# Bonus of the first two chunks through TensorE, the state update behind the values, decay copies on ScalarE

## What is computed

```python
cur = np.einsum('bhd,bhe->bhde', u[None] * kt, vt)
y[:, :, t] = np.einsum('bhd,bhde->bhe', rt, state + cur)
state = wt[:, :, :, None] * state + np.einsum('bhd,bhe->bhde', kt, vt)
```

## Time and profile before

| | |
|---|---|
| median of three runs | 666.23 us |
| the profiled execution | 666.1 us, of which 664.3 us are the traced span |
| TensorE busy | 655.3 us (99%), 4683 matmuls |
| VectorE, ScalarE, GpSimd busy | 402.5, 218.3, 243.1 us |
| chain that ended last | 90% TensorE |
| granted TensorE clock | full in every slice of the page |
| first real product of the dense layer (step 0) | 19.95 us |

### The profile page before, as it was taken

How to read it: one execution, slowest core, us unless ns; L and a number is a source line. 1 busy time by engine, 2 the same in 40 slices (tenths; PEclk the granted TensorE clock), 3 DMA queues, 4 the chain that set the end, 5 groups by cost and what they waited for, 6 DMA issues and landing times.

```text
span 664.3 us, 12577 instructions
## 1 busy us (share of the span) xinstructions
PE 655.3 (99%) x4683; PEld 600.0 (90%) x4683; DVE 402.5 (61%) x750; ACT 218.3 (33%) x447; POOL 243.1 (37%) x293
## 2 busy tenths in 40 slices
PE   9999999999999999999999999999999999999998
PEld 6888899877878888899999999999999999999997
DVE  7888888766644333656565656565656565656563
ACT  3673434434335444422222222222222222222221
POOL 4888332222014069996006940008920009000000
PEclk9999999999999999999999999999999999999999
DMA  9913322220000032300002200003200011001011
GB/s 338 405 78 126 107 104 86 84 84 1 1 1 1 4 95 92 96 1 1 1 1 95 96 1 0 0 5 104 83 1 0 0 48 49 0 1 47 0 48 48
DMA packets 12862, 38.81 MB, mean 58 GB/s; under 512 B 1552, under 2 KB 3344, under 8 KB 12816
## 3 DMA queue, kind: packets, MB, share of 16 engines
q1 hardware_dynamic: 12528, 37.77, 16.4%
q10 hardware_dynamic: 288, 0.39, 0.2%
HBM read 35.80 MB, written 2.36 MB: 57 GB/s over the span
## 4 chain that ended last, share of the span: by engine, by line
PE 90%; DVE 6%; ACT 1%; issue 1%; POOL 0%; DMA 0%; DVEq 0%; ACTq 0%; POOLq 0%
PE bank L1029 29%; PE bank L1030 28%; PE bank L1031 28%; PE bank L919 2%; DVE fr L628 1%; DVE fr L636 1%; PE bank L976 1%; PE bank L945 1%; DVE w_lo L720 1%; PE bank L931 1%; PE bank L988 1%; DVE bank L755 0%; DMA rkw<-rkw_dram 0%; DVE x_lo L712 0%; DVE g_lo L761 0%
## 5 line engine op out<-in xcount | busy, mean ns | idle before, releaser
L1029 PE MATMUL bank<-x_lo,w_hi 128*128 128x256 f32 (+2 forms) x432 | 146.9, 340 | 1.7 <-DVE x_lo L712 0.9
L1031 PE MATMUL bank<-x_hi,w_hi 128*128 128x256 f32 (+2 forms) x432 | 143.3, 332 | 0.0
L1030 PE MATMUL bank<-x_hi,w_lo 128*128 128x256 f32 (+2 forms) x432 | 143.2, 331 | 0.0
L1030 PE MATMUL bank<-w_hi,g_lo 128*128 128x384 f32 x384 | 129.6, 338 | 0.0
L1031 PE MATMUL bank<-w_hi,g_hi 128*128 128x384 f32 x384 | 129.3, 337 | 0.0
L1029 PE MATMUL bank<-w_lo,g_hi 128*128 128x384 f32 x384 | 129.0, 336 | 0.0
L581 ACT ACTIVATE g_hi<-bank 128x512 fp32r<-128x512 f32 x96 | 57.6, 600 | 144.2 <-DVE bank L850 122.2
L1029 PEld LDWEIGHTS bank<-x_lo,w_hi 128*128 128x128 f32 x432 | 81.2, 188 | 13.0 <-issue 1.8
L1031 PEld LDWEIGHTS bank<-x_hi,w_hi 128*128 128x128 f32 x432 | 81.2, 188 | 9.0
L1030 PEld LDWEIGHTS bank<-x_hi,w_lo 128*128 128x128 f32 x432 | 81.3, 188 | 8.2
L417 POOL TENSOR_TENSOR raw<-raw 128x128 f32<-128x128 f32 x16 | 7.5, 467 | 200.5 <-DMA raw<-w_dram 200.5
(11 more groups left out here) (98 smaller groups left out, 1134.4 us busy)
## 6 DMA issues: line engine op xcount, KB each, us to landing
raw<-w_dram SPq DMA_DIRECT2D x48, 384.0 KB, 3.8
rkw<-rkw_dram SPq DMA_DIRECT2D x10, 772.5 KB, 4.5
tok<-tok_dram SPq DMA_DIRECT2D x12, 576.0 KB, 4.1
out_dram<-acc SPq DMA_DIRECT2D x10, 192.0 KB, 1.9
rkw<-rkw_dram SPq DMA_DIRECT2D x2, 512.0 KB, 4.5
rkw<-rkw_dram SPq DMA_DIRECT2D x2, 260.5 KB, 3.4
out_dram<-acc ACTq DMA_DIRECT2D x2, 192.0 KB, 2.0
u_rep<-u_dram SPq DMA_DIRECT2D x1, 192.0 KB, 6.3
```

Of the source, the lines that this page charges most:

```text
L1029: pe.matmul(out, wh, ml, start=start, stop=False, skip_group_check=shared)
L1030: pe.matmul(out, wl, mh, start=False, stop=False, skip_group_check=shared)
L1031: return pe.matmul(out, wh, mh, start=False, stop=stop, skip_group_check=shared)
```

## The change

For chunks 0 and 1 the token form of r and k is not loaded. ScalarE copies the unscaled k (d by token) into the unused part of `tok` and writes r·u into `ru`, four activations of 128 columns with a column of u as scale. GpSimd (chunk 0) and VectorE (chunk 1) multiply the two, and TensorE sums over d by four matmuls of 128 columns of weights with a two-column matrix of ones. VectorE multiplies v by these sums for both chunks. `scale_k` and `scale_r` of the two chunks now wait for ScalarE's copies. The column form of u (`u_col`) is loaded by two DMAs of single floats, ahead of the second chunk's decays; u by row moves behind the first eight slices.

`update(c)` of chunks from 2 on moves to the end of step 4c+2, behind the values, with its sums in bank 7; `add_update(c)` moves into step 4c+3, ahead of `scale_r(c+1)`. The scores of a chunk now wait for the update of the chunk before. The `tail` copy goes to ScalarE. At the start `turn_bonus(0)` moves ahead of `update(0)`, and `lo_w(0, 1)` behind both `lo_x`.

```diff
+TAILS = ALPHAS | {FIRST: INVERSES[FIRST] + 1}
-        BESIDE = dict(x=bank[6:8], yt=bank[5], kt=bank[5], u=heads_in(bank[5], 0))
+        BANKS0 = dict(x=bank[6:8], ..., bonus=bank[3])
+        BESIDE = dict(x=bank[6:8], yt=bank[5], kt=bank[5], u=heads_in(bank[7], 256))
 @block.sync
             load_decays(0)
             load_rk(0)
+            sp.wait_ge(s_zero, 1)
+            for o in range(2):
+                u_heads = bass.AP(u_d.tensor, o * D, [[1, D], [PD, PAIRS]])
+                sp.dma_start(u_col[64 * o:64 * o + D, :], u_heads, ...).then_inc(s_uc, 16)
             load_decays(1)
...
-            load_tok(0)
+            load_v(0)
+            load_v(1)
+            load_slices(0, 1, 2, 3, 4, 5, 6, 7)
             sp.dma_start(u_rep[:, :], u_d).then_inc(s_u, 16)
 @block.gpsimd
             pool.wait_ge(s_f, FIRST)
+            pool.wait_ge(s_kc, 1)
+            pool.wait_ge(s_ru, PAIRS)
+            pool.tensor_tensor(ru[:, 0, :], ru[:, 0, :], kc_of(0), ALU.mult).then_inc(s_ruk[0], 1)
             pool.wait_ge(s_qp, FIRST)
-            ... (the products of r, k, u and bonus_v of the first two chunks)
 @block.scalar
+            def copy_tail(c):
+                act.wait_ge(s_f, c + 1)
+                need(act, s_al, c - 1)
+                act.copy(tail[:, c % 2, :], fr[:, 2 * SEG - 1:SCAN:2 * SEG]).then_inc(s_tail, 1)
+            def raw_rk(c):
+                act.wait_ge(s_rkw[c], 16)
+                act.copy(kc_of(c), k_of(c)).then_inc(s_kc, 1)
+                act.wait_ge(s_uc, 32)
+                for p in range(PAIRS):
+                    cols = slice(p * CH, (p + 1) * CH)
+                    act.activation(ru[:, c, cols], q_of(c)[:, cols], ACT.Copy, scale=u_col[:, p:p + 1]).then_inc(s_ru, 1)
+            copy_tail(0)
+            raw_rk(0)
+            raw_rk(1)
+            copy_tail(1)
             copy_kt(0, BANKS0)
 @block.vector
             scale_r(1)
-            dve.tensor_tensor(tok[0][:, 0:DM], tok[0][:, 0:DM], u_rep[:, :], ALU.mult).then_inc(s_ru, 1)
-            bonus(0)
+            dve.tensor_tensor(ru[:, 1, :], ru[:, 1, :], kc_of(1), ALU.mult).then_inc(s_ruk[1], 1)
+            bonus_v(0, BANKS0)
             mask_scores(1, 0, BANKS1)
             mask_scores(1, 1, BANKS1)
-            bonus(1)
-            bonus_v(1)
+            bonus_v(1, BANKS1)
             lo_w(0, 0)
-            lo_w(0, 1)
             lo_x(0, BANKS0["yt"])
             lo_x(1, BANKS1["yt"])
+            lo_w(0, 1)
...
-                for c in due(n, 4):
-                    if c < NUPDATE:
-                        add_update(c, BESIDE)
                 elu(n)
...
+                for c in due(n, 3):
+                    if c < NUPDATE:
+                        add_update(c, BESIDE)
                 for c in due(n, 0, PRODUCTS):
 @block.tensor
 scores:         pe.wait_ge(s_x, FIRST)
+                    pe.wait_ge(s_sum, 2 * min(c, NUPDATE))
 update:
-                if banks is BESIDE:
-                    pe.wait_ge(s_x, c + 1)
+            def bonus(c, banks):
+                pe.wait_ge(s_ruk[c], 1)
+                if c == 1:
+                    pe.wait_ge(s_kt, 1)
+                for p in range(PAIRS):
+                    ins = pe.matmul(banks["bonus"][:, 2 * p:2 * p + 2], ru[:, c, p * CH:(p + 1) * CH], ones[:, :],
+                                    start=True, stop=True)
             fill(3, 1)
+            bonus(0, BANKS0)
             fill(1, 2)
             values(0, BANKS0["yt"])
             fill(5, 1)
             scores(1, BANKS1)
+            bonus(1, BANKS1)
             turn_k(1, BANKS1)
+            turn_bonus(0, BANKS0["yt"], False)
             update(0, BANKS0)
             fill(1, 4)
             values(1, BANKS1["yt"])
-            turn_bonus(0, BANKS0["yt"], False)
             turn_bonus(1, BANKS1["yt"], False)
...
                     values(c, BESIDE["yt"])
-                for c in due(n, 3):
                     if c < NUPDATE:
                         update(c, BESIDE)
```

More of the change, by code:

```diff
@@ L134, in bass_linear_attention_elu_ffn_dense_experts @@
             u_rep = sb("u_rep", [P, DM], scope=scope)
+            u_col = sb("u_col", [P, PAIRS], scope=scope)
+            ones = sb("ones", [P, 2], scope=scope)
+            ru = sb("ru", [P, FIRST, NRK], scope=scope)
             bonus_sb = sb("bonus_sb", [P, 2, H], scope=scope)
@@ L164, in heads_in @@
             return b[:, first:first + PAIRS * D]
-        BANKS0 = dict(x=bank[6:8], yt=bank[2], kt=bank[5], u=heads_in(bank[6], 0))
-        BANKS1 = dict(x=bank[0:2], yt=bank[4], kt=bank[7], u=heads_in(bank[7], 0))
-        BESIDE = dict(x=bank[6:8], yt=bank[5], kt=bank[5], u=heads_in(bank[5], 0))
+        BANKS0 = dict(x=bank[6:8], yt=bank[2], kt=bank[5], u=heads_in(bank[6], 0), bonus=bank[3])
+        BANKS1 = dict(x=bank[0:2], yt=bank[4], kt=bank[7], u=heads_in(bank[7], 0), bonus=bank[5])
+        BESIDE = dict(x=bank[6:8], yt=bank[5], kt=bank[5], u=heads_in(bank[7], 256))
         s_const = sem("s_const")
@@ L186, in bass_linear_attention_elu_ffn_dense_experts @@
         s_rk = sem("s_rk")
+        s_uc = sem("s_uc")
+        s_kc = sem("s_kc")
         s_ru = sem("s_ru")
+        s_ruk = [sem(f"s_ruk{i}") for i in range(FIRST)]
+        s_pb = sem("s_pb")
         s_bon = sem("s_bon")
@@ L282, in rk_done, with kc_of @@
         def rk_done(c):
-            return 3 + 4 * (c - 1)
+            return 4 * (c - 1)
+        def kc_of(c):
+            return tok[c][:, 0:NRK]
         def column_halves(first):
@@ L338, in load_rk, with load_v @@
                 sp.dma_start(rkw[c][:, 0:2 * NRK], rkw_d[c][:, 0:2 * NRK]).then_inc(s_rkw[c], 16)
+            def load_v(c):
+                sp.dma_start(tok[c][:, 2 * DM:3 * DM], tok_d[c][:, 2 * DM:3 * DM]).then_inc(s_tok[c], 16)
             load_decays(0)
             load_rk(0)
+            sp.wait_ge(s_zero, 1)
+            for o in range(2):
+                u_heads = bass.AP(u_d.tensor, o * D, [[1, D], [PD, PAIRS]])
+                sp.dma_start(u_col[64 * o:64 * o + D, :], u_heads, allow_slow_non_contiguous=True).then_inc(s_uc, 16)
             load_decays(1)
@@ L371, in _ @@
         def _(pool):
+            pool.memset(u_col[:, :], 0.0).then_inc(s_zero, 1)
             pool.memset(st[:, :, :, :], 0.0).then_inc(s_zero, 1)
@@ L376, in _ @@
             pool.memset(v_odd[:, :, :, :], 0.0).then_inc(s_zero, 1)
+            pool.memset(ones[:, :], 0.0).then_inc(s_zero, 1)
+            for o in range(2):
+                pool.wait_ge(s_zero, 6 + o)
+                pool.memset(ones[64 * o:64 * o + D, o:o + 1], 1.0).then_inc(s_zero, 1)
+            pool.wait_ge(s_zero, 8)
             pool.memset(credit[:, 2:3], 0.0).then_inc(s_down, RING)
@@ L566, in _ @@
                     copy_odd(c)
+                for c in due(n, 1, TAILS):
+                    copy_tail(c)
                 if n % J1 == LAG - 1 and n > LAG:
@@ L641, in alphas @@
             def alphas(c):
[L643 to L649, removed]
+                first_half = fr[:, SEG - 1:SCAN:2 * SEG]
+                need(dve, s_st, c - 3)
+                dve.wait_ge(s_tail, c - 1)
+                dve.tensor_tensor(alpha[:, c % 2, :], tail[:, c % 2, :], first_half, ALU.mult).then_inc(s_al, 1)
             def scale_k(c):
@@ L654, in scale_k @@
                 landed(dve, s_rkw, c)
+                if c < FIRST:
+                    dve.wait_ge(s_kc, c + 1)
                 dve.tensor_tensor(halves(k_of(c)), halves(k_of(c)), factors(0, SCAN + SEG + 1),
@@ L693, in bonus, with bonus_v @@
             def bonus(c):
[L695 to L699, removed]
+                dve.wait_ge(s_rk, rk_done(c))
+                dve.wait_ge(s_cv, c - 1)
                 dve.tensor_reduce(bonus_sb[:, c % 2, :], tok[c % DEEP][:, 0:DM].rearrange("p (h d) -> p h d", h=H),
                                   AX.X, ALU.add).then_inc(s_bon, 1)
-            def bonus_v(c):
-                dve.wait_ge(s_bon, c + 1)
+            def bonus_v(c, banks):
+                dve.wait_ge(s_pb, c + 1)
+                landed(dve, s_tok, c)
                 dve.tensor_tensor(bonus_v_sb[:, c % 2, :].rearrange("p (h e) -> p h e", h=H),
                                   v_of(c).rearrange("p (h e) -> p h e", h=H),
-                                  bonus_sb[:, c % 2, :].unsqueeze(2).broadcast_to([P, H, D]),
+                                  banks["bonus"][:, 0:H].unsqueeze(2).broadcast_to([P, H, D]),
                                   ALU.mult).then_inc(s_cv, 1)
@@ L926, in turn_k @@
                     pe.wait_ge(s_x, c)
-                    pe.wait_ge(s_sum, 2 * c)
                 k = k_of(c)
@@ L962, in turn_bonus @@
                     pe.wait_ge(s_x, c)
-                    pe.wait_ge(s_sum, 2 * min(c, NUPDATE))
                 for k in range(KT):
@@ L1012, in _ @@
             fill(3, 1)
+            pe.wait_ge(s_zero, 8)
+            bonus(0, BANKS0)
             fill(1, 2)
```

31 lines of the change are left out of this document (11 added, 20 removed).

## The result

The changed kernel takes 667.94 us (median of 10 executions, 667.89 to 668.33), the kernel before beside it 666.17 (10 executions, 666.01 to 666.51). The ratio is 1.0027, with a 95% interval of 1.0018 to 1.0035: 1.77 us slower. The profiled execution took 667.93, with a span of 666.1 us where before it was 664.3. The forecast was 667.1.

The account below looks back on a forecast made before the run. TensorE, busy 99% of the span, was taken as the bound, with ScalarE and VectorE pacing the first steps. Start +2.3 and chunks -1.3 gave +1.0 on 666.1, so 667.1 us, range 664.0 to 669.4.

Parts of the forecast that it names:

- `u_col`, 0.2 late: Start: the single-float loads land at 5.9 us, ScalarE's activations end at 7.1, so `scale_r(0)` starts 0.2 us late.
- Rival C: Start: `u_col` lands two microseconds behind 5.9, everything behind it goes later, total 669.1 us; chance 0.14.
- The bonus, 0.9 each: Start, TensorE: eight loads of 128 columns per bonus, 0.11 us from one to the next, 0.9 us taken.
- Rival E: Start: a bonus costs only 0.2 us, loads following at 0.026; start +0.9, total 665.7 us; chance 0.14.
- The start, +2.3: Before step 0: TensorE's list with both bonuses and the moved `lo_w(0, 1)` make step 0 2.3 us later, at 22.2.
- The moved half of `lo_w`: End of the start, VectorE: `lo_w(0, 1)`, 0.9 us, becomes the last thing `slice_ready(0)` waits for.
- The shift carried in full through the first tile: Step 0 to 38.69 us: the ScalarE and VectorE loop sets the pace unchanged, so step 0's delay passes through whole.
- The chunks, -1.3: Chunks 2 to 9: moved update and tail copy save 1.3 us net, though chunks 5 and 6 lose 0.5 each.
- 0.35 us less per chunk: Chunks 2 to 9, TensorE: update between values and `up` needs no switch from wide products and back, saving 0.35 us each.
- c2's 0.8: Chunk 2: a tail copy of 0.53 us and the longest wait, 0.9, go; gain 0.8 us.
- B: Chunks 2 to 9: VectorE keeps up and the update move gains 4.0 us, total 663.3 us; chance 0.20.
- D: 256-token tiles: `scale_r` behind `add_update` is late in every chunk, chunks +0.8 us, total 669.2 us; chance 0.11.

Follow-up runs that it names:

- run 6: The changed kernel with one fill instead of five ahead of `scores(1)`: 667.42 us.
- run 7: The changed kernel with `bonus(0)` moved behind `values(0)` and one fill instead of five ahead of `scores(1)`: median 667.47 us, executions scattered from 666.72 to 669.83.
- run 5: The changed kernel with `lo_w(0, 1)` put back ahead of both `lo_x` in the start: 667.50 us.
- run 10: The changed kernel with GpSimd held before `lo_w(1)` in the start until VectorE's `bonus_v(1)` is done: 668.41 us.
- run 8: The kernel before with tail copies on ScalarE, the update moved and `scale_r` one step earlier, its start and bonus kept: 663.97 us.
- run 11: The changed kernel with GpSimd's products for the bonus of chunk c held until `scale_r(c-1)` is done: 667.47 us.
- run 4: The changed kernel with `scale_r` one step earlier for chunks from 3 on: 665.89 us.
- run 2: The kernel before with the update move alone, `add_update` placed as in the change: 666.24 us, ratio 1.0000.

## Why the prediction came out as it did

The time lay in the range. It had 667.1, of which the start was 2.3 and the chunks -1.3. Measured: 2.2, and -0.4 for first tile and chunks. The difference is over the 0.2% bound (0.27%, interval 0.18 to 0.35), so it falls to the slower side, to which 0.38 was given. That the time came within 0.9 us is in part luck: the chunks missed by 1.3 us, and 0.4 of that was given back by the first tile, for which the sum had nothing.

**`u_col`, 0.2 late: it was 0.** The two loads landed 3.3 and 3.4 us after their issue, quicker than that of r and k ahead of them (3.6), and the last activation ended at 6.8. There was no room left: the second load landed at about 5.5, and the first activation began at 5.54. An activation took 0.385 us where 0.29 was reckoned, but they follow each other 0.3 apart and began at 5.54. Rival C is refuted. Its landing, two microseconds behind 5.9, was also half a microsecond past the prediction's own late end of 7.4. The rule of one descriptor per element, from the Trainium skill ("DMA: Bandwidth & Descriptors", Rules for kernel authors), spoke for the late end; 384 single floats in 3.4 us show no price here.

**The bonus, 0.9 each: right.** Eight loads of 128 columns in 0.97 us, though only two columns move. Rival E is refuted: it is 0.11 us from one to the next. The Trainium skill ("TensorE: Matmul & The Clock Gate", Wait — 56ns, not 53.3ns?) states its 25 ns as a floor that the distance never goes below. The rows don't contradict that; reading the floor as the price is what fails.

**The start, +2.3: right to 0.1, with each step in its place, though two sizes cancelled.** `scores(1)` at 14.22 (14.2), `hi_x(1)` at 20.48 (20.3), step 0 at 22.16 (22.2) behind `lo_w(0, 1)`. Runs 6 and 7 show that TensorE's list was the cause of the 1.17 up to `scores(1)`. The moved half of `lo_w` was reckoned at 0.9 as the last thing awaited; it lasted 0.55 and run 5 shows that its place costs 0.44. Most of what this left over `hi_x(1)` had used up by coming 0.2 late. For `scores(1)` at 13.05 the prediction had a loss of 1.6; run 7 has 1.04.

**The shift carried in full through the first tile: wrong by 0.37.** "GpSimd starts its `w_lo` work earlier; it wasn't waited for" was true, yet it paid (run 10): the engine was a neighbour, not a releaser.

**The chunks, -1.3: here the sum failed, it was -0.03.** The failed term is "0.35 us less per chunk" for the switches. `update` behind the values has a gap of 0.20 us of its own (eight of them, in the rows above), so the move saves one switch, 0.17 or 0.18 in each of c7 to c9, and not 0.35 to 0.5. That is 0.8 of the 1.3. In c2 0.44 came of the 0.8, as the scores of chunk 3 now waited for `scale_r`. What was right: c5 and c6 lose 0.56 and 0.53 (0.5 each), c3 and c4 lie within 0.05 of their terms. And the mechanism of c5 is as described: `add_update` ahead of `scale_r`, five waits of 0.7 at most. Inside it two tenths cancelled: `scale_r` took 0.93 instead of the 1.1 reckoned, and `elu` came about 0.2 later.

**Not seen at all: what each part does alone.** The tail copy was reckoned as a piece of c2's 0.8. It is the one part of the change that helps, 1.1 us, and it gives all of this without the update move. The prediction priced the two as one and so could not say that the update move costs 1.1 where the tail copies are in.

**Rivals.** B (the update move pays) failed as the change stands, and run 8 shows the condition under which it holds: `scale_r` out of its way. D had the waits right, in all five chunks, and c2 with its 0.4, but not the price of c3 and c4 (0.5 lost each; measured -0.15 and -0.01), since the update's old wait was gone in the same chunks.

## What to carry to other kernels

Look at what stands in an engine's list ahead of the instruction that is awaited: a wait of a consumer (`update` for `x_lo`) can be closed by moving a 0.5 us copy to another engine or by reordering the consumer, and the two don't add. Work moved in front of the awaited instruction opens the next wait, so a reorder on one engine is tried together with its partner on the other (`update` and `scale_r`, on top of the tail copies: +1.1 and +3.7 alone, -1.1 together). A reduction that TensorE does "for free" costs its weight loads (0.11 us for one of 128 columns, 0.026 for one of 32) wherever TensorE's own list sets the pace. And where a VectorE instruction on the path has two operands in SBUF (the on-chip memory), look at what GpSimd has just begun beside it.

## What the runs showed of the hardware

- Multiplying on GpSimd beside a VectorE product of two SBUF operands lengthens the latter: `scale_r` 0.69 us alone, 0.93 in the changed kernel and 1.13 before, with run 11 as proof of the cause for the 0.93. The Trainium skill ("SBUF — State Buffer", SBUF: two separate sides) says that such an instruction with two SBUF inputs contends with a GpSimd operation that reads SBUF, and that the second fully blocks until the first is done. The rows agree, the full block included. Beside the `scale_r` at 97.17 in the changed kernel, GpSimd's timeline and its single durations (ns, min/median/max) are

```profile
96.95 1.59 POOL L412 TENSOR_TENSOR tok<-tok 128x192 f32<-128x192 f32 x2
```
```profile
L412 POOL TENSOR_TENSOR tok<-tok x2: 597/818/1039, 97.0 to 97.5; 128x192 f32<-128x192 f32 x2
```

  The first took 0.60 and ended at 97.55; `scale_r` ended at 98.10, 0.55 later. The second began at 97.51 and took 1.04, to 98.55, 0.45 after the end of `scale_r`: each ends a fixed time behind the other's end, and its row counts the waiting as its own time. In the kernel before, the neighbour in chunk 5 is not a product but `bonus_v`, which began ahead of the `scale_r` at 94.56:

```profile
94.31 0.83 POOL L394 TENSOR_TENSOR bonus_v_sb<-tok,bonus_sb 128x384 f32<-128x384 f32 x1 [9.50 <-DVE bonus_sb L700]
```

  It ended at 95.15, and `scale_r` ended at 95.69, again 0.55 later; run 4's `scale_r` of 1.09 us does the same (66.72 and 67.27). So 0.93 and 1.13 are not two speeds of one instruction but the remainder of the neighbour plus 0.55.
- The same makes a start late by chance. In the profiled execution of run 2 the tokens landed 0.9 us later than in the kernel before, so that GpSimd's product began just ahead of VectorE's last scan of the start instead of well before it:

```profile
10.39 1.00 POOL L462 TENSOR_TENSOR tok<-tok 128x384 f32<-128x384 f32 x1 [7.62 <-DMA tok<-tok_dram]
```

  The scan (`inverses(1)`, L636, from 10.45) took 2.04 instead of 1.23, and step 0 came 0.83 late. It ended 1.10 behind the product's end (12.49 and 11.39), about its own length less 0.14, as the 0.55 is for the 0.69 of `scale_r`.
- Two loads of 192 single floats each landed 3.3 and 3.4 us after issue. Behind them the load of r and k of chunk 1 was issued at 3.57 instead of 2.60 and landed at 7.8, where it had landed at 7.9.
- In run 7 single executions came out up to 3 us longer than the fastest, in part with a lower mean granted clock. Four fills were out of the start there; in run 6, which took out as many, all lay within 1 us, so the fills alone are not shown to be the cause.
